# A gated scan with an ELU feed-forward: the matmuls of blocks 1 to 11 walk their 512 columns in ten other orders

## The reference

```python
sig = 1.0 / (1.0 + np.exp(-f_logit))
f = lower_bound + (1.0 - lower_bound) * sig
i = 1.0 - f
for t in range(S):
    h = f[:, t] * h + i[:, t] * x[:, t]
    y[:, t] = h
...
h = y.reshape(B * S, D) @ w_in
g = np.where(h > 0.0, h, np.exp(np.minimum(h, 0.0)) - 1.0)
out = g @ w_out
```

## Time and profile before

| What | Value |
|---|---|
| Median of 2 runs | 989.69 us (989.53 to 989.86) |
| Span of the profiled execution | 987.9 us |
| TensorE, records of matmuls | 983.2 us, 4362 matmuls |
| TensorE, weight loads | 817.7 us, 4362 loads |
| ScalarE | 791.6 us, 1424 instructions |
| VectorE | 726.4 us, 916 instructions |
| GpSimd | 633.2 us, 477 instructions |
| Granted TensorE clock | 1.000 of full |

### The profile page before, as it was taken

One profiled execution on the slowest core, in us unless ns is written; L12 is line 12 of the kernel. 1 busy time (PEld: TensorE's weight loads), 2 busy tenths in 40 slices (PEclk: granted clock), 3 DMA queues, 4 the chain that ended last, 5 costly groups with the idle time before them and its releaser, 6 DMA issues.

```text
span 987.9 us, 15016 instructions
## 1 busy us (share of the span) xinstructions
PE 983.2 (100%) x4362; PEld 817.7 (83%) x4362; DVE 726.4 (74%) x916; ACT 791.6 (80%) x1424; POOL 633.2 (64%) x477
## 2 busy tenths in 40 slices
PE   9999999999999999999999999999999999999998
PEld 6998888888888888888888888888888888888887
DVE  6987876976886796697688679678768867956444
ACT  7988878878888887877887887888788788787775
POOL 2588796576567558557656756856765765675444
PEclk9999999999999999999999999999999999999999
DMA  7212012002102201200210210120021021001001
GB/s 265 66 33 91 0 35 63 33 1 76 54 1 60 69 1 42 64 21 10 65 53 0 64 63 0 51 66 10 25 61 42 0 74 53 0 0 45 1 1 43
DMA packets 23078, 42.02 MB, mean 43 GB/s; under 512 B 2560, under 2 KB 4096, under 8 KB 23040
## 3 DMA queue, kind: packets, MB, share of 16 engines
q1 hardware_dynamic: 22752, 41.10, 12.9%
q10 hardware_dynamic: 288, 0.46, 0.1%
HBM read 29.10 MB, written 12.45 MB: 42 GB/s over the span
## 4 chain that ended last, share of the span: by engine, by line
PE 100%; DVE 0%; POOL 0%; issue 0%; POOLq 0%
PE acc L886 17%; PE acc L888 17%; PE acc L887 17%; PE h L859 14%; PE h L855 14%; PE h L857 14%; PE h L992 1%; PE h L993 1%; PE h L991 1%; PE h L999 1%; PE h L958 0%; PE h L968 0%; PE acc L991 0%; PE acc L992 0%; PE acc L993 0%; PE acc L958 0%
## 5 line engine op out<-in xcount | busy, mean ns | idle before, releaser
L327 POOL TENSOR_TENSOR g_lo<-e,g_hi 128x512 fp32r<-128x512 f32 (+1 forms) x384 | 519.4, 1363 | 348.6 <-ACT g_hi L471 347.7
L457 ACT ACTIVATE e<-h 128x512 f32<-128x512 f32 (+1 forms) x379 | 225.6, 595 | 151.7 <-PE h L859 129.2
L710 DVE SCALAR_TENSOR_TENSOR e<-e,h 128x512 f32<-128x512 f32 (+1 forms) x379 | 256.3, 676 | 70.7 <-ACT e L463 70.4
L887 PE MATMUL acc<-g_lo,w_out_hi 128*128 128x512 f32 (+1 forms) x768 | 297.2, 387 | 0.0
L886 PE MATMUL acc<-g_hi,w_out_hi 128*128 128x512 f32 (+1 forms) x768 | 297.2, 387 | 0.0
L888 PE MATMUL acc<-g_hi,w_out_lo 128*128 128x512 f32 (+1 forms) x768 | 297.2, 387 | 0.0
L463 ACT ACTIVATE e<-e 128x512 f32<-128x512 f32 (+1 forms) x384 | 241.5, 629 | 9.6 <-issue 1.2
L471 ACT CAST g_hi<-e 128x512 fp32r<-128x512 f32 (+1 forms) x384 | 232.4, 605 | 16.9 <-DVE e L710 16.9
L859 PE MATMUL h<-a_hi,w_in_lo 128*128 128x512 f32 x616 | 239.7, 389 | 0.0
L855 PE MATMUL h<-a_hi,w_in_hi 128*128 128x512 f32 x616 | 239.7, 389 | 0.0
L857 PE MATMUL h<-a_lo,w_in_hi 128*128 128x512 f32 x616 | 239.6, 389 | 0.0
(11 more groups left out here) (77 smaller groups left out, 563.0 us busy)
## 6 DMA issues: line engine op xcount, KB each, us to landing
opening<-forget_logit SPq DMA_DIRECT2D x44, 256.0 KB, 2.6
x<-value SPq DMA_DIRECT2D x44, 256.0 KB, 2.7
out<-out_sb SPq DMA_DIRECT2D x44, 256.0 KB, 2.0
w_in_raw<-w_in SPq DMA_DIRECT2D x8, 256.0 KB, 6.1
w_out_raw<-w_out SPq DMA_DIRECT2D x8, 256.0 KB, 6.8
out<-out_sb SPq DMA_DIRECT2D x4, 224.0 KB, 1.9
x<-value SPq DMA_DIRECT2D x3, 224.0 KB, 6.6
opening<-forget_logit SPq DMA_DIRECT2D x2, 224.0 KB, 6.6
```

The source lines that it names most:

```text
L327: nc.gpsimd.tensor_tensor(g_lo[:, t % RING, 0:w], e[:, t % TILES, 0:w], g_hi[:, t % RING, 0:w].bitcast(F32), ALU.subtract).then_inc(g_lo_r ...
L457: nc.scalar.activation(e[:, i, 0:w], bank_of(j, t)[:, 0:w], ACT.Relu, scale=-1.0).then_inc(r_ready, 1)
L710: nc.vector.scalar_tensor_tensor(e[:, t % TILES, 0:w], e[:, t % TILES, 0:w], -1.0, bank_of(j, t)[:, 0:w], ALU.add, ALU.max).then_inc(g_rea ...
L887: nc.tensor.matmul(bank, hi, g_lo[:, t % RING, 0:w], start=False, stop=False)
```

## The change

A table `STYLES` gives each of five groups of blocks a pair of orders, the first for the rounds 0 to 3 and the second for the rounds 4 to 7 of a block. An order is four numbers: turns, run, and two flags. `in_order` reads the 512 columns as b groups of `turns` runs of `run` columns. The walk takes in each turn one run from every group; the last two flags walk the turns, or the groups, downwards. Within a run the columns always ascend. With (4, 4, 0, 0), for example, the columns come as 0 to 3, 16 to 19, 32 to 35, ..., and then 4 to 7, 20 to 23, and so on.

Both the columns that are read and the columns of PSUM that are written are walked in this order, so that each result stands where it stood. Block 1 has the first pair, block 2 the second, the odd blocks 3 to 9 the third, the even blocks 4 to 10 the fourth, and block 11 the fifth. Tiles of the block before that are multiplied in a block's first rounds take the order of those rounds. The matmuls of block 0, those of its last tiles in block 1, and the tail have no order.

```diff
+STYLES = (((8, 4, 0, 0), (8, 2, 0, 0)), ((4, 16, 0, 0), (2, 16, 0, 0)), ((4, 4, 0, 0), (4, 4, 1, 1)),
+          ((4, 4, 1, 0), (4, 4, 0, 1)), ((4, 8, 0, 0), (2, 4, 1, 1)))
...
+def in_order(columns, style):
+    if style is None:
+        return columns
+    turns, run, turns_down, runs_down = style
+    steps = columns.rearrange("p (b a c) -> p a b c", a=turns, c=run)
+    if turns_down:
+        steps = steps[:, ::-1]
+    return steps[:, :, ::-1] if runs_down else steps
...
-            def product(j, par, q, k, bank, start=False):
+            def product(j, par, q, k, bank, style, start=False):
                 w = width(j)
                 hi, lo = w_in_hi[:, q, k], w_in_lo[:, q, k]
                 a_h, a_l = a_parts(par, k)
-                nc.tensor.matmul(bank[:, 0:w], hi, a_h[:, 0:w], start=start, stop=False,
-                                 skip_group_check=True)
-                nc.tensor.matmul(bank[:, 0:w], hi, a_l[:, 0:w], start=False, stop=False,
-                                 skip_group_check=True)
-                return nc.tensor.matmul(bank[:, 0:w], lo, a_h[:, 0:w], start=False, stop=True,
-                                        skip_group_check=True)
-
-            def second(j, t, half):
+                into = in_order(bank[:, 0:w], style)
+                a_h, a_l = in_order(a_h[:, 0:w], style), in_order(a_l[:, 0:w], style)
+                nc.tensor.matmul(into, hi, a_h, start=start, stop=False, skip_group_check=True)
+                nc.tensor.matmul(into, hi, a_l, start=False, stop=False, skip_group_check=True)
+                return nc.tensor.matmul(into, lo, a_h, start=False, stop=True, skip_group_check=True)
+
+            def second(j, t, half, style=None):
...
                 bank = acc[:, b, half, 0:w]
-                nc.tensor.matmul(bank, hi, g_hi[:, t % RING, 0:w], start=opens, stop=False)
-                nc.tensor.matmul(bank, hi, g_lo[:, t % RING, 0:w], start=False, stop=False)
-                done = nc.tensor.matmul(bank, lo, g_hi[:, t % RING, 0:w], start=False, stop=closes)
+                g_h, g_l = g_hi[:, t % RING, 0:w], g_lo[:, t % RING, 0:w]
+                if not first:
+                    bank, g_h, g_l = in_order(bank, style), in_order(g_h, style), in_order(g_l, style)
+                nc.tensor.matmul(bank, hi, g_h, start=opens, stop=False)
+                nc.tensor.matmul(bank, hi, g_l, start=False, stop=False)
+                done = nc.tensor.matmul(bank, lo, g_h, start=False, stop=closes)
...
-            def whole(j, par):
+            def whole(j, par, styles):
                 def m(q, back, i, half):
 
                     at = q - back
                     if at >= 0:
-                        second(j, TILES * at + i, half)
+                        second(j, TILES * at + i, half, styles[q // 4])
                     else:
-                        second(j - 1, TILES * (PAIRS + at) + i, half)
+                        second(j - 1, TILES * (PAIRS + at) + i, half, styles[q // 4])
...
-                    product(j, par, q, P1, trunk(q), start=True).then_inc(p1_done, 1)
+                    product(j, par, q, P1, trunk(q), styles[q // 4], start=True).then_inc(p1_done, 1)
...
-            whole(1, 1)
-            whole(2, 0)
+            whole(1, 1, STYLES[0])
+            whole(2, 0, STYLES[1])
             with nc.Fori(1, (BLOCKS - 2) // 2, engines=(mybir.EngineType.PE,),
                          hint_back_edge=True) as i:
-                whole(2 * i + 1, 1)
-                whole(2 * i + 2, 0)
+                whole(2 * i + 1, 1, STYLES[2])
+                whole(2 * i + 2, 0, STYLES[3])
             j = BLOCKS - 1
-            whole(j, 1)
+            whole(j, 1, STYLES[4])
```

More of the change, by code:

```diff
@@ L916, in whole @@
                     pe.wait_ge(g_ready, TILES * (n - 1) + C12 + 1)
-                    product(j, par, q, P5, h[:, 2], start=True).then_inc(p5_done, 1)
+                    product(j, par, q, P5, h[:, 2], styles[q // 4], start=True).then_inc(p5_done, 1)
                     m(q, 2, C21, 0)
@@ L922, in whole @@
                     pe.wait_ge(fork_ready, n - PAIRS + 1)
-                    product(j, par, q, P2, h[:, 3]).then_inc(c11_ready, 1)
+                    product(j, par, q, P2, h[:, 3], styles[q // 4]).then_inc(c11_ready, 1)
                     if q == 0:
                         pe.wait_ge(a_lo_ready[P6], low_count(j, P6))
-                    product(j, par, q, P6, trunk(q)).then_inc(p6_done, 1)
+                    product(j, par, q, P6, trunk(q), styles[q // 4]).then_inc(p6_done, 1)
                     m(q, 1, C11, 0)
@@ L932, in whole @@
                     pe.wait_ge(u4_ready, n - PAIRS + 1)
-                    product(j, par, q, P3, h[:, 2]).then_inc(c12_ready, 1)
+                    product(j, par, q, P3, h[:, 2], styles[q // 4]).then_inc(c12_ready, 1)
                     if q == 0:
                         pe.wait_ge(a_lo_ready[P7], low_count(j, P7))
-                    product(j, par, q, P7, trunk(q)).then_inc(p7_done, 1)
+                    product(j, par, q, P7, trunk(q), styles[q // 4]).then_inc(p7_done, 1)
                     m(q, 1, C12, 1)
@@ L942, in whole @@
                     pe.wait_ge(c22_ready, n + 1)
-                    product(j, par, q, P4, trunk(q)).then_inc(c21_ready, 1)
+                    product(j, par, q, P4, trunk(q), styles[q // 4]).then_inc(c21_ready, 1)
             def plain_weights(unit, half):
```

## The result

The changed kernel takes 1038.56 us (median of two runs, 1038.03 to 1039.09) against 989.69 before: a ratio of 1.0493, 95% interval [1.0472, 1.0514], 48.9 us slower. The prediction was 989.7 with a range up to 1035, so the time lies above it.

A forecast was written before the change was run, and what follows sets the result against it. TensorE's pace from one matmul to the next was taken as the bound: from 80.78, 3960 x 226.67 ns = 897.6 us plus 6.1 end at 984.5; the store closes 987.9, the median lies 1.8 over: 989.7. Range 945 to 1035.

The forecast's parts named there:

- a hand-over of some 14 ns once stream and load are both through: In each matmul step, at 512 and 448 columns: a hand-over of some 14 ns after column stream and weight load end.
- I take nil: Price of a jumping stream in the 3930 reordered matmuls: nil, the step stays at 226.67 ns; chance 0.55.
- rival of the falling extra: Reordered matmuls: the extra 13.3 ns a step falls, 951.6 us, or 937.3 with all of it gone; chance 0.17.
- slower in one place: Second half of block 1: runs of 2 columns are too short, 16.8 to 38.4 us more, 1006 to 1028; chance 0.12.
- rival of the jumps: Blocks 1 to 11: one tick for each new 64-byte stretch entered, 142.8 us in all, 1132.5; chance 0.12.
- the 13.3 ns: Part of each 226.67 ns matmul step beyond the 213.3 ns that 512 columns take at 2.4 GHz.

## Why the prediction was wrong

- **What bounds the kernel** was right, and so was the count: 3930 matmuls, 3.93 us for each ns of the step.
- **The step that failed** is "a hand-over of some 14 ns once stream and load are both through", and with it "I take nil". Two widths and a load of 188 ns fitted one formula, and I took the fit for a cause. A third width refutes it (188.1 ns at 416 columns), and moving the weights by 128 bytes refutes it again (232.4 ns with nothing else changed). The widths of 496 and 488 show in their place an extra that isn't fixed. The reason named for the rival of the falling extra, the weights that are read at the same time, has the runs on its side: moving them moves the step. That rival's price was of the right kind as well: one order of the ten is faster, at 220.0 ns, and used everywhere it gains 25.8 us. In the changed kernel it had one half, 1.2 us.
- **The rival "slower in one place"** was the main event, at the upper end of its price: 180 x 204.4 ns = 36.8 us, within 16.8 to 38.4. Its reason holds in a sharper form: not the run but the visit to 16 bytes counts. I gave it 0.12, though the argument for it, that this one order uses half of 16 bytes at a time, needed nothing but a limit on visits.
- **The rival of the jumps** (one tick for each new 64-byte stretch) is wrong in kind: (4, 4) orders jump 128 times and step by 223.4 to 232.8 ns, not 266.7; and block 2, where it saw nothing, lost 4.7 us.
- **The range** ended at 1035, 3.6 us too low, because each rival stood alone. The half in one place (+36.8) and the other orders (+11 net) added up, as ten orders in one program can. The ends should have been sums over the halves. A figure beside the sum was off too: blocks 3 to 10 take 652.8 us before (16 halves of 40.80), not 660.
- **The rules of the Trainium skill.** The Trainium skill, PSUM — Partial Sum Buffer, Specifications, gives PSUM lines of 8 bytes and says that any pattern that isn't contiguous slows matmuls significantly. Here it didn't: with writes in the ten orders each full half stayed at 40.80 us (runs of a single column were not tried). The Trainium skill, Advanced Engine Details and Errata, SBUF Cachelines, asks for at least two hits on a line of 16 bytes. Here, with 4-byte columns at the full clock, two columns a visit gave half the rate (431 to 461 ns), and four gave the usual one. The Trainium skill, TensorE: Matmul & The Clock Gate, Step-by-step: what each phase is for, says that the loads have a read port of their own and don't take bandwidth from the running matmul. The run with the weights 128 bytes later disagrees: 23 us more with the same instructions.

Open stays how the reads share SBUF in detail: which part of the address decides, how much of the 13.3 ns the loads make, and why (4, 8, 0, 0) alone of the 22 orders in turns gets 220 ns, while the same runs walked downwards don't.

## What to carry to other kernels

Where TensorE is full and its steps are longer than columns over clock, look at the addresses: measure the step between starts, move weights against data by 64 or 128 bytes (here the place they had was already the best of those tried), and try a few orders of the moving columns, ten to a kernel, then the best one alone, since a stretch can depend on the one ahead of it. Use up each 16 bytes of a 4-byte operand in one visit. And when a change mixes several variants, add their cases up before stating a range.

## What was not expected of the hardware

- The same code can have two paces. In the changed kernel the steps of (4, 4, 0, 0) went through cycles of several matmuls, and the same loop code took 40.80 us in block 3 and 40.22 in block 5. (4, 8, 1, 0) took 42.70 in block 5 and 41.98 in block 7, and (4, 8, 0, 0) 41.51 us behind a half with shifted weights where it takes 39.60 behind itself. One reading is that how a stretch begins sets how it goes on, for at least 180 matmuls; no run was made to test it.
- Writes to PSUM in runs of 2 to 16 columns with 8 to 64 columns from run to run cost nothing: 989.56 us against 989.78.
- Moving the weights by 256 bytes against the data is neutral to 0.1%, by 128 bytes it costs 2.3%.
